# Second layer: a new order of each engine's work in a step, the cosine's intermediate in PSUM, and a new opening for the first four chunks

## What is computed

```
state = 0                                   # per batch (4) and head (8), 48 x 48
for t in range(768):                        # attention with a decaying state
    state = alpha[t][:, None] * state + outer(k[t], v[t]);   y[t] = q[t] @ state
x = y as 3072 tokens x 384
h = x @ w_in;   x = (h * tanh(softplus(h))) @ w_out      # first layer, 384 -> 2048 -> 384
h = x @ w2_in;  out = (h * cos(h)) @ w2_out              # second layer, same sizes
```

## Time and profile before

| | |
|---|---|
| median of 3 runs | 970.9 us (970.53 to 972.66) |
| the profiled execution | 970.7 us, its span 969.0 us |
| PE busy | 916.2 us (95%) |
| DVE, ACT, POOL busy | 484.5, 415.4, 359.4 us |
| DMA, mean over the span | 50 GB/s |

### The profile page before, as it was taken

The page is one execution under the profiler, slowest core; times in us unless marked ns, Lnnn a source line. Parts: engine busy times, 40 slices in busy tenths (PEclk is TensorE's granted clock), DMA queues, the critical chain, the costliest instruction groups (busy, mean ns, idle before and its releaser), DMA issues.

```text
span 969.0 us, 14130 instructions
## 1 busy us (share of the span) xinstructions
PE 916.2 (95%) x5550; PEld 742.3 (77%) x5550; DVE 484.5 (50%) x622; ACT 415.4 (43%) x697; POOL 359.4 (37%) x288
## 2 busy tenths in 40 slices
PE   7699999999999999999999997997997997998996
PEld 6588888888888888888887875885885885886784
DVE  7633223323233222310217767776777676677664
ACT  1253332223223223223556555555555555555453
POOL 6475434433334433432554222222223222223222
PEclk7899999999999999999999998998999999999899
DMA  7545321122112122100332001001001000100000
GB/s 196 147 123 135 90 68 37 36 56 84 37 37 69 44 64 69 28 1 33 115 98 83 1 0 66 1 1 57 10 0 33 34 0 4 62 1 0 33 1 32
DMA packets 17153, 48.13 MB, mean 50 GB/s; under 512 B 2752, under 2 KB 2752, under 8 KB 17088
## 3 DMA queue, kind: packets, MB, share of 16 engines
q1 hardware_dynamic: 17088, 47.23, 16.9%
HBM read 37.79 MB, written 9.44 MB: 49 GB/s over the span
## 4 chain that ended last, share of the span: by engine, by line
PE 57%; DVE 27%; ACT 10%; issue 3%; POOL 1%; DMA 0%; POOLq 0%; ACTq 0%; DVEq 0%
PE bank L378 25%; PE bank L397 24%; DVE shared L615 11%; DVE shared L613 6%; DVE g L621 5%; ACT shared L494 5%; ACT shared L496 5%; PE bank L315 3%; DVE shared L611 3%; PE bank L333 2%; PE bank L340 1%; PE bank L345 1%; PE bank L309 1%; PE bank L353 1%; POOL shared L704 0%
## 5 line engine op out<-in xcount | busy, mean ns | idle before, releaser
L691 POOL TENSOR_TENSOR g_lo<-g,g_hi 128x512 fp32r<-128x512 f32 x192 | 249.0, 1297 | 521.6 <-ACT g_hi L473 521.6
L397 PE MATMUL bank<-g_hi,w_hi 128*128 128x512 f32 x576 | 233.1, 405 | 34.6 <-ACT x_out L467 21.0
L397 PE MATMUL bank<-g_lo,w_hi 128*128 128x512 f32 x576 | 228.3, 396 | 0.0
L397 PE MATMUL bank<-g_hi,w_lo 128*128 128x512 f32 x576 | 228.1, 396 | 0.0
L473 ACT ACTIVATE g_hi<-g 128x512 fp32r<-128x512 f32 x192 | 121.2, 631 | 131.0 <-PE bank L397 105.9
L378 PE MATMUL bank<-x_hi,w_hi 128*128 128x512 f32 x576 | 168.3, 401 | 0.0
L397 PEld LDWEIGHTS bank<-g_hi,w_hi 128*128 128x128 f32 x576 | 109.7, 191 | 72.0 <-ACT g_hi L473 23.4
L378 PE MATMUL bank<-x_hi,w_lo 128*128 128x512 f32 x576 | 164.8, 395 | 0.0
L378 PE MATMUL bank<-x_lo,w_hi 128*128 128x512 f32 x576 | 162.8, 391 | 0.0
L615 DVE SCALAR_TENSOR_TENSOR shared<-shared 128x512 f32<-128x512 f32 x96 | 142.4, 1483 | 3.3
L494 ACT ACTIVATE shared<-shared 128x512 f32<-128x512 f32 x96 | 60.7, 632 | 170.4 <-DVE shared L615 170.4
(11 more groups left out here) (63 smaller groups left out, 584.4 us busy)
## 6 DMA issues: line engine op xcount, KB each, us to landing
w_raw<-w_in SPq DMA_DIRECT2D x32, 384.0 KB, 3.2
shared<-aqk_in SPq DMA_DIRECT2D x44, 192.0 KB, 3.6
v_sb<-v_in SPq DMA_DIRECT2D x24, 256.0 KB, 4.2
shared<-aqk_in SPq DMA_DIRECT2D x48, 96.8 KB, 3.8
mid<-x_out SPq DMA_DIRECT2D x6, 768.0 KB, 3.8
shared<-mid SPq DMA_DIRECT2D x6, 768.0 KB, 5.5
out<-x_out SPq DMA_DIRECT2D x5, 768.0 KB, 4.0
out<-x_out SPq DMA_DIRECT2D x3, 256.0 KB, 2.4
```

Of the source, the lines that this page charges most:

```text
L397: mm = nc.tensor.matmul(acc[m][:, :], wp[:, f, cols], gp[:, tile % GB, :], start=(f == 0 and n == 0), stop=(f == FT - 1 and n == 2))
L691: nc.gpsimd.tensor_tensor(g_lo[:, tile % GB, :], g[:, tile % GB, :], g_hi[:, tile % GB, :].bitcast(F32), ALU.subtract).then_inc(glo_ready, 1)
```

## The change

Three things. In layer 2 each engine's order in a step changes: ACT goes from `cosine(s-1)`, `turns(s)`, `g_part(s-1)` to `turns(s)`, `g_part(s-2)`, `cosine(s-1)`; DVE from `gate(s-1)`, `reduce_angle(s)` to `reduce_angle(s)`, `gate(s-1)`; POOL does `g_rest(s-2)` for `g_rest(s-1)`; and `second_product` waits for g_lo only at the first matmul that reads it. The value between L613 and L615 goes to PSUM bank 7. In layer 1 all chunk work is one step later. And the opening is written anew: loads, warm matmuls, the scans of chunk 4, the zeroing of the state (now on ACT), and the banks of the first four updates.

```diff
 def update_of(c):
-    at = c * PAIRS * D if c < 2 else 0
-    bank = banks[(3, 3, 5, 6)[c]] if c < BATCH else banks[5]
+    at = c % 2 * PAIRS * D if c < BATCH else 0
+    bank = banks[3 + c // 2] if c < BATCH else banks[5]
...
 # SP, opening (step() uses chunk_at(s, 3) for chunk_at(s, 2))
             load_a(0)
             load_qk(0)
-            load_v(0)
             load_a(1)
             load_qk(1)
-            load_v(1)
+            load_v(0)
             load_a(2)
             load_qk(2)
-            load_v(2)
+            load_v(1)
             load_a(3)
             load_qk(3)
             load_w(0)
+            load_v(2)
             load_w(1)
+            load_a(4)
             load_v(3)
+            load_qk(4)
             load_w(2)
             load_w(3)
-            load_a(4)
-            load_qk(4)
             load_v(4)
...
 # PE
-                if c >= BATCH and before < UPDATES:
+                if c > BATCH and before < UPDATES:
                     pe.wait_ge(sum_ready, 2 * c)
...
                 pe.wait_ge(ghi_ready, tile + 1)
-                pe.wait_ge(glo_ready, tile + 1)
                 if tile == 0:
-                    pe.wait_ge(sum_ready, 4)
+                    pe.wait_ge(sum_ready, 2 * BATCH)
...
+                        if m == 0 and gp is g_lo:
+                            pe.wait_ge(glo_ready, tile + 1)
...
-            warm(14)
+            warm(20)
             scores(0)
-            warm(3)
+            warm(4)
             scores(1)
-            warm(2)
             values(0)
             warm(2)
             scores(2)
             values(1)
-            warm(2)
             scores(3)
             values(2)
-            warm(4)
             values(3)
-            warm(4)
...
 # ACT, step(); keep_x_hi moves from chunk_at(s, 2) to (s, 3), keep_keys from (s, 0) to (s, 1)
-                if alive(s - 1) and s - 1 >= TILES:
-                    cosine(s - 1)
                 if alive(s - 1) and s - 1 < TILES:
                     g_part(s - 1)
...
                         turns(s)
+                if alive(s - 2) and s - 2 >= TILES:
+                    g_part(s - 2)
                 if alive(s - 1) and s - 1 >= TILES:
-                    g_part(s - 1)
+                    cosine(s - 1)
...
 # DVE
-                dve.wait_ge(upd_done, c + 1)
+                dve.wait_ge(upd_done, c + 1 if c >= BATCH else c // 2 * 2 + 2)
...
+                part = banks[7][:, :]
...
-                nc.vector.scalar_tensor_tensor(tn, un, -C1, h, ALU.mult, ALU.add).then_inc(rr_ready, 1)
+                nc.vector.scalar_tensor_tensor(part, un, -C1, h, ALU.mult, ALU.add).then_inc(rr_ready, 1)
                 dve.wait_ge(rr_ready, n + 1)
-                nc.vector.scalar_tensor_tensor(tn, un, -C2, tn, ALU.mult, ALU.add).then_inc(w_ready, 1)
+                nc.vector.scalar_tensor_tensor(tn, un, -C2, part, ALU.mult, ALU.add).then_inc(w_ready, 1)
...
+                if alive(s) and s >= TILES:
+                    reduce_angle(s)
                 if alive(s - 1) and s - 1 >= TILES:
                     gate(s - 1)
-                if alive(s) and s >= TILES:
-                    reduce_angle(s)
...
             keep_x_lo(2)
+            keep_x_lo(3)
             split_w(1)
-            keep_x_lo(3)
+            grow(4)
             for c in range(BATCH):
                 add_state(c)
-            grow(4)
             split_w(3)
...
 # POOL
-                if alive(s - 1):
-                    g_rest(s - 1)
+                back = 2 if s - 2 >= TILES else 1
+                if alive(s - back) and (s - back < TILES) == (back == 1):
+                    g_rest(s - back)
...
-            for c in range(3):
+            for c in range(BATCH):
                 prepare(c)
-            nc.gpsimd.memset(state[:, :, :, :], 0.0).then_inc(state_zero, 1)
-            prepare(3)
             split_w(0)
+            prepare(4)
             split_w(2)
-            prepare(4)
```

More of the change, by code:

```diff
@@ L237, in step @@
             def step(s):
-                c = chunk_at(s, 2)
+                c = chunk_at(s, 3)
                 if c is not None and c + 2 < CHUNKS:
@@ L408, in step @@
                     second_product(s - LAG)
-                c = chunk_at(s, 0)
+                c = chunk_at(s, 1)
                 if c is not None:
@@ L525, in _ @@
             act.preload_act_table_set("mish")
+            act.wait_ge(const_ready, 2)
+            nc.scalar.activation(state[:, :, :, :].rearrange("p b a e -> p (b a e)").rearrange(
+                "p (n t) -> p n t", t=P), ident[:, None, :].to_broadcast([P, BATCH * PAIRS * 2 * D // P, P]),
+                ACT.Copy, scale=0.0).then_inc(state_zero, 1)
             keep_keys(0)
@@ L638, in step @@
                     split_w(piece)
-                c = chunk_at(s, 1)
+                c = chunk_at(s, 2)
                 if c is not None and c + 1 < CHUNKS:
                     grow(c + 1)
-                c = chunk_at(s, 0)
+                c = chunk_at(s, 1)
                 if c is not None:
```

## The result

The changed kernel took 907.9 us, the median of four runs (905.5 to 908.8), against 970.7 us for the kernel before: a ratio of 0.935, with an interval of 0.932 to 0.937. The prediction was 905.5, in a range of 901 to 913.

A forecast was written before the change was run, and what follows sets the result against it. PE bounds layer 1, a 4.63 us ring across ACT and DVE bounds layer 2. 510.16 - 9 (opening) + 388.2 (layer 2) + 9.7 (tail) + 4.5 = 903.6 span, + 1.7 + 0.2 = 905.5 us; range 901 to 913.

The forecast's parts named there:

- Both predicted waits of PE in the tail: Tail: PE loses 0.65 us waiting for g_lo(190), then waits from 7.2 to 7.95 for g_lo of tile 191.
- the term of 9: Opening: a gain of 9 us, taken between 7.4 at least and 11.2 at best.
- the best case: Opening: the clock no longer falls in the idle time ahead of 10.37; second product 0 at 45.0, a gain of 11.2.
- the prediction's lower bound: Opening: scores(4) 3.05 us earlier, 0.4 saved on warm matmuls, low clock kept; second product 0 at 48.8, gain 7.4.
- 2 us less: Opening: by the skill's clock rule the warm matmuls help, and the sum is the best case, 2 us less.
- The price of L615: Layer 2, DVE's second subtraction: 1.50 us with both sources in SBUF, 0.69 with one in PSUM.
- upper bound: Layer 2, first subtraction writing to PSUM: at most 1.50 us, L615's own time; 0.69 taken, 0.42 the lower bound.
- The 0.9 us that it drew from that section for the tail: Tail: by the skill's larger fixed cost for a PSUM source, the sum would end about 0.9 us later.
- The new order alone would be enough: Layer 2: the new order brings it to PE's 4.08 us a tile with L615 unchanged; PSUM adds 0.8 us of air.
- The waits that the others named: Opening, late raw pieces or POOL's order: 4 to 8 us, chance 0.10; layer 2 block ends still stopping: 20 us, 0.06.
- The rival on the other side: Layer 2: first subtraction to PSUM dear, kernel slower from 2.8 us on, about 988 at 3.0; chance 0.03.
- the ring: Layer 2 before: Abs, Sin, gate and reduction wait on each other across ACT and DVE, 4.63 us against PE's 4.08.

The follow-up runs named there:

- the changed kernel's second profile: The changed kernel run again, unaltered, and profiled: median 906.8 us, ratio 0.934, the profiled execution 908.0 us.
- the better kernel: The changed kernel with layer 2's old order of ACT, DVE and POOL, and warm matmuls filling PE's opening gaps: 901.5 us, ratio 0.929.

## Why the prediction was right, and where it was not

**Layer 2: right in all that carries the sum.** Step 4.08, with 388.3 from the first `turns` to the end of first_product(191) for 388.2; the write to PSUM 0.70 for 0.69; no stop at block ends but the first, 0.28 for 0.6; the tail 9.7 (first_product(191) ends at 889.62, the last matmul at 899.34), 4.5 behind it. Both predicted waits of PE in the tail are there, listed with 0.32 and 0.25, less than the 0.65 and 0.75 reckoned; g_lo of the last tile comes at 7.8 for 7.95, and that sets the end.

**The opening: the term of 9 was mis-sized by about 2.** The profiled execution has 8.98, and its clock is what the best case asked for at 12 to 16. That it meets the 9 is luck: it is the shortest of four, the other three are 1.6 to 3.3 longer, and it is the only profile in which the clock held behind the 2.03 us ahead of scores(3). By medians the opening alone gives 5 to 7; in the traces second product 0 comes 7.5 earlier in the kernel with the opening alone and 6.5 in the changed kernel's second profile. That is about the prediction's lower bound (7.4). The step that failed is "I take 9, between the two, as no row decides on the clock". It asked for the clock at one gap, the one ahead of 10.37. PE has three gaps of some 2 us in the new opening, ahead of the scores of chunks 0, 3 and 4, and each can lower the clock behind it: the first costs 0.7 us where it does, the second 1.4 to 1.6, and filling the third gave 1.9 to 2.2. The second fell in seven profiles of eight and the third, unfilled, in all. That accounts for 907.9 against 905.5 as far as it is known: only two of this kernel's eight executions were profiled. The best case needed all three filled, and then came (45.1). The rule that the prediction set beside this term, from the Trainium skill's page TensorE: Matmul & The Clock Gate (What's actually happening), that the clock falls after idle time and rises after sustained work, agrees in its direction with the filled gap (1.9 us less). The "2 us less" that the prediction drew from it did not come, since two gaps were left.

**The price of L615: right number, wrong cause.** The prediction laid 1.50 against 0.69 on where the operands lie. The run of the order alone shows the same operation, both sources in SBUF, at 0.69 while POOL is idle, and ending 0.55 us behind POOL's operation in the 95 cases where the two overlap. So 1.50 was no upper bound either (1.99). With one source in PSUM it takes 0.69 with POOL's subtraction beside it (L617 at 601.81, POOL from 601.18 to 602.48), and so all 96 times. The Trainium skill has this, in SBUF — State Buffer (Who interferes with whom): DVE's second pair of SBUF ports is GpSimd's own, and is held by one of them at a time. The trace agrees. The prediction cited another section, on the fixed cost of a source in PSUM, which says nothing of POOL; this one would have given a reason for the 0.69 that it took. The 0.9 us that it drew from that section for the tail did not come: the tail took 9.7, as summed.

**What each half does: half seen.** "The new order alone would be enough" holds (914.9 beside 914.3 for both). That PSUM alone would also be (912.3) lay in the prediction's own numbers, 4.63 less 0.81 against 4.08, and was not drawn from them. It is what led to the better kernel.

**The rivals.** The waits that the others named are not in the trace: raw pieces 2 and 3 kept ACT waiting for 2.02 and 0.50 us, hidden from PE, and PE didn't stop at block ends but for 0.28 at the first. The rival on the other side had its point about right: at 2.9 us for the first subtraction the kernel is slower than before. By the rival's sum 2.9 gives about 978 (970.9 - 9 + 95 x 0.17), near the 981.7 measured, but partly by luck: it reckoned a step of 4.8, where the step is 4.57, and left out what DVE does beside the step.

## What to carry to other kernels

Where an engine's operations follow each other across queues, add up the ring: it holds the kernel only while its sum is above the slowest engine's own step, so either a new order or one shorter member can free it, and a second cure on top brings nothing and may lengthen the tail. Before a slow instruction is replaced, look at what the other engines do at that moment: if its end always lies the same time behind the end of another engine's operation, it waits for that one. Here, moving one source of the subtraction to PSUM ended its wait for POOL. When one profiled execution holds a stretch whose clock can go either way, price that stretch from the runs' medians, look at every gap of PE in it and not at one, and try filling them.

## What the runs showed of the hardware that was not expected

- DVE's second subtraction, 512 columns with two SBUF sources, took 0.69 us alone and up to 1.99 beside a POOL operation; in all 95 such cases of the run of the order alone it ended 0.54 to 0.56 us after POOL's. With one of its sources in PSUM it kept 0.69 in all 96.
- The rounding on DVE (L613 in the changed kernel) has a single source, in SBUF, and was not safe from POOL: it met a POOL operation three times. It took 1.68 us at 515.02, where POOL was already splitting weights (from 514.58 to 516.42), and 0.42 at 511.51 and 519.54, where POOL started just after it; POOL's 1.30 were then 1.40 and 1.53. The second profile of the changed kernel shows the same three.
- The same idle time of 2.03 us was followed by a granted clock of 1.00 over 26 to 28 in one profile and of 0.50 to 0.59 in seven. Behind the gap ahead of 10.38 the clock over 12 to 14 was 0.51 after 2.31 us of idle time and 1.00 after 2.02. The two places together were worth most of the 2.5 us between two executions of the changed kernel. With all gaps filled the clock was 1.00 from 2 to 47 in both kernels that did so.
- A DVE step that was 0.5 us above PE's made layer 2 take 0.74 more per tile, since the copies and splits on DVE were no longer covered.
